# Whole expert tiles in each round of the loop, a wait for hT_hi first in the second product, and one quarter of a weight split moved from GpSimd to VectorE

## The chip, the cores and the metric

The kernel runs on one core of one Trainium2 chip. The metric is the device time of one execution in microseconds (us), the median of several runs; lower is better.

## The reference

Three layers follow one another, all in float32, on 4 batches of 576 tokens with 512 features.

```python
attn = softmax_d(q) @ (softmax_s(k)^T @ v)          # linear attention, 8 heads of 64
u    = x + (relu(x^T @ w_tok1) @ w_tok2)^T          # token mixer, 576 -> 256 -> 576
x1   = u + relu(u @ w_ch1) @ w_ch2                  # channel mixer, 512 -> 1536 -> 512
e[s] = argmax(x1[s] @ w_gate) if s == 0 or sigmoid(x1[s] @ w_local) < 0.5 else e[s-1]
out[s] = p[e[s]] * (relu(x1[s] @ w1[e[s]]) @ w2[e[s]])   # one of 8 experts, 512 -> 1024 -> 512
```

`p` is the softmax over the eight gate logits.

## The kernel before

**Products.** Every large product is made of three: a float32 matrix is kept as a high part (float32r) and a low part (raw minus high), and TensorE adds high x high, high x low and low x high into one PSUM bank (`SPLIT`). So weights have to be split before use: ScalarE or GpSimd writes the high part (`ACTIVATE` or `CAST`), VectorE or GpSimd subtracts it from the raw weights for the low part. The same holds for activations: ScalarE copies a PSUM bank to the high part (`u_h`, `hid_h`, `hT_h`, `xgT_h`), then VectorE subtracts (`u_l`, `hid_l`, `hT_l`, `xgT_l`).

**Front.** The order on each engine is written out by hand. TensorE warms up with small products (`keep_warm`), does attention of batch 0, then the eight tiles `u_tile(0, j)` (L603 on), each of eight products of 128x288 in bank 4 or 5; tile j waits until VectorE has finished `u_l` of tile j-2 (`u_done`). Behind them come the chunks of the channel mixer, `chunk(0, idx)`: twelve `hid` chunks and four `y` chunks for each half of the batch, with two banks in turn, so chunk idx waits for VectorE's result of chunk idx-2. In the first `hid` chunk `first_ready(j)` waits for the low part of quarter j of the first channel weights (`wc1`, four quarters of 128 rows, each split in two halves of 768 columns).

Who makes the low parts of `wc1`: VectorE quarters 0 and 2 (`split_first`, L1551, called between the `u_out` steps), GpSimd quarters 1 and 3 (L1861). The second channel weights (`wc2`, twelve pieces of 512 columns) are split by VectorE (even pieces, L1556) and GpSimd (odd pieces, L1864), ScalarE making the high parts in order (L1060).

**Experts.** The last batch's tokens are routed, and tokens are grouped by expert into tiles of 128 rows. Tiles 0 to 3 belong to the commonest expert and are written out one by one; the rest run in a loop over tiles `EARLY` (4) to `n`, with `n` known only on the chip. Of a tile t:

- GpSimd gathers its rows (`gather`), `x_turn(t)` transposes them on TensorE (four transposes, L743), ScalarE and VectorE make `xgT`.
- `hidden(t, n, half)` is twelve products of 128x512 (L803) into bank 0 or 1; ScalarE applies relu into `hs` (L1123).
- `h_turn(t, half)` is four transposes (L815) into bank 2 or 3; ScalarE makes `hT_h` (L1127) and signals `hT_hi`, VectorE makes `hT_l` (L1717) and signals `hT_done`.
- `output(t, n, half)` is twelve products (L828) into bank 5. VectorE scales the result (`yo_out`, L1728), GpSimd scatters it to the output.

A round of TensorE's loop before is `h_turn(t,0)`, `x_turn(t+1)`, `hidden(t,1)`, `output(t,0)`, `h_turn(t,1)`, `hidden(t+1,0)`, `output(t,1)`. It therefore straddles two tiles: `hidden(4,0)` stands ahead of the loop, and the last round also does `hidden` half 0 of a tile past the end. `output` waits for `hT_done` before its first product. Which slot holds a tile's weights is read in the loop (`version_of`, a load from `table`, L834).

While an expert is in use, the next expert's weights (eight units: 0 to 3 of `w1`, 4 to 7 of `w2`) are loaded by SyncE's queue and split by ScalarE (high, L1003) and VectorE (low, L1701), in places of a round that a word of bits picks (`units(..., FIRST_HALF | SECOND_HALF | AT_END | AFTER_END, ...)`).

```python
for a, x in SPLIT:                    # L827, in output: high x high, high x low, low x high
    last = pe.matmul(bank[5][:, :], hT[a][:, f, :], w2s[x][...], ...)
```

## Time and profile before

| | us |
|---|---|
| median of 3 runs | 725.35 (725.33 to 726.04) |
| profiled execution | 725.15 |
| its span, first to last instruction | 723.0 |
| TensorE products (PE), busy | 711.3 |
| TensorE weight loads (PEld), busy | 647.4 |
| VectorE (DVE), busy | 306.9 |
| ScalarE (ACT), busy | 231.8 |
| GpSimd (POOL), busy | 143.7 |

The page of the profile gives the time in which each engine works. Products overlap, and a product's end is modelled, so the starts of neighbouring products say more than their durations. "Idle before" a row is the time in which its engine had nothing to do, with the instruction that released it. Some instructions of TensorE's sequencer (PEldq) are listed as well: branches, loads into registers and address arithmetic, which run ahead of the array.

### The profile page before, as it was taken

The page shows a single profiled execution, that of the slowest core. Times are in us where ns is not written, and L with a number is a line of the kernel's source. Part 1 is how long each engine was busy: PE and PEld are TensorE (multiplying, and loading weights), DVE is VectorE, ACT ScalarE, POOL GpSimd, SP SyncE. Part 2 cuts the span into 40 slices and gives each one's busy share as a digit, 9 for nine tenths or more (in the row PEclk, how much of TensorE's full clock was granted, in tenths as well). Part 3 has the DMA queues.
Part 4 walks back from the last instruction along what each step waited for, and adds up shares of the span by engine and source line. Part 5 has one row for each costly group of instructions (what it writes and reads, how often), then busy time and mean ns, then how long its engine had stood idle before and what let it go on. Part 6 is the DMA issues. An engine that isn't in the chain of part 4 may idle for free.

```text
span 723.0 us, 14218 instructions
## 1 busy us (share of the span) xinstructions
PE 711.3 (98%) x4936; PEld 647.4 (90%) x4937; DVE 306.9 (42%) x639; ACT 231.8 (32%) x451; POOL 143.7 (20%) x174
## 2 busy tenths in 40 slices
PE   7999999999999999999999999999999999999997
PEld 7889999999999999999999999788888888888885
DVE  5775232235232235232225723785545552222631
ACT  4653142023142023142021133321536442222621
POOL 7754020002020002020000015022321312121311
PEclk9999999999999999999999999999999999999999
DMA  9952131012131012100010350114844561010000
GB/s 238 351 122 67 34 100 34 1 35 67 34 100 34 1 35 66 34 34 1 1 39 1 117 164 15 54 44 136 281 160 150 186 224 58 23 58 23 34 21 12
DMA packets 72013, 57.65 MB, mean 80 GB/s; under 512 B 54908, under 2 KB 57244, under 8 KB 71968
## 3 DMA queue, kind: packets, MB, share of 16 engines
q1 hardware_dynamic: 68448, 47.58, 22.1%
q0 software_dynamic: 3520, 9.44, 3.9%
q8 instruction: 32, 0.52, 0.3%
q14 instruction: 13, 0.11, 0.0%
HBM read 48.79 MB, written 10.31 MB: 82 GB/s over the span
## 4 chain that ended last, share of the span: by engine, by line
PE 96%; DVE 2%; POOL 0%; ACT 0%; issue 0%; POOLq 0%; DVEq 0%
PE bank L658 42%; PE bank L803 16%; PE bank L828 16%; PE bank L586 5%; PE bank L620 3%; PE bank L815 3%; PE bank L612 2%; PE bank L689 2%; PE bank L743 1%; PE bank L574 1%; PE bank L558 1%; PE bank L530 1%; PE bank L597 1%; DVE wc_l L1551 1%; PE bank L666 1%; PE bank L544 0%
## 5 line engine op out<-in xcount | busy, mean ns | idle before, releaser
L658 PE MATMUL bank<-u_h,wc_h 128*128 128x288 f32 x384 | 117.2, 305 | 0.1
L658 PE MATMUL bank<-hid_h,wc_h 128*128 128x288 f32 x384 | 115.0, 299 | 0.0
L658 PE MATMUL bank<-hid_l,wc_h 128*128 128x288 f32 x384 | 113.2, 295 | 0.0
L658 PE MATMUL bank<-u_h,wc_l 128*128 128x288 f32 x384 | 113.1, 295 | 0.0
L658 PE MATMUL bank<-u_l,wc_h 128*128 128x288 f32 x384 | 113.1, 294 | 0.0
L658 PE MATMUL bank<-hid_h,wc_l 128*128 128x288 f32 x384 | 113.1, 294 | 0.0
L803 PE MATMUL bank<-wslots,xgT_h 128*128 (+1 forms) x344 | 110.6, 402 | 0.0
L828 PE MATMUL bank<-wslots,hT_h 128*128 (+1 forms) x336 | 104.2, 391 | 0.0
L1509 DVE SCALAR_TENSOR_TENSOR hid_l<-bank,hid_h 128x288 fp32r<-128x288 f32 x96 | 43.5, 455 | 107.9 <-ACT hid_h L1009 106.7
L1009 ACT ACTIVATE hid_h<-bank 128x288 fp32r<-128x288 f32 x96 | 39.2, 409 | 113.4 <-PE bank L658 113.0
L828 PEld LDWEIGHTS bank<-wslots,hT_h 128*128 128x128 f32 x336 | 62.6, 188 | 13.3 <-DVE hT_l L1717 0.5
L658 PEld LDWEIGHTS bank<-u_h,wc_h 128*128 128x128 f32 x384 | 72.1, 188 | 1.0 <-DVE hid_l L1509 0.3
L658 PEld LDWEIGHTS bank<-u_l,wc_h 128*128 128x128 f32 x384 | 72.2, 188 | 0.1
L658 PEld LDWEIGHTS bank<-hid_h,wc_l 128*128 128x128 f32 x384 | 72.3, 188 | 0.0
L658 PEld LDWEIGHTS bank<-hid_l,wc_h 128*128 128x128 f32 x384 | 72.1, 188 | 0.1
L658 PEld LDWEIGHTS bank<-hid_h,wc_h 128*128 128x128 f32 x384 | 72.0, 188 | 0.1
L658 PEld LDWEIGHTS bank<-u_h,wc_l 128*128 128x128 f32 x384 | 72.0, 188 | 0.0
L803 PEld LDWEIGHTS bank<-wslots,xgT_h 128*128 128x128 f32 x344 | 61.4, 189 | 11.3
L803 PE MATMUL bank<-wslots,xgT_l 128*128 (+1 forms) x172 | 67.7, 394 | 0.0
L828 PE MATMUL bank<-wslots,hT_l 128*128 (+1 forms) x168 | 65.6, 391 | 0.0
L1516 DVE TENSOR_TENSOR x1T<-bank,u_h 128x288 f32<-128x288 f32 x32 | 14.6, 457 | 115.3 <-PE bank L658 115.3
L1915 POOL DMA_INDIRECT out_dram<-yo,id_out x21 | 22.8, 1084 | 172.7 <-DVE yo L1728 172.7
(270 smaller groups left out, 1055.3 us busy)
## 6 DMA issues: line engine op xcount, KB each, us to landing
w1raw<-in_moe_w_dram SPq DMA_DIRECT2D x20, 512.0 KB, 5.2
w2raw<-in_moe_w_dram SPq DMA_DIRECT2D x20, 512.0 KB, 3.6
wc_raw<-in_moe_w_ch_dram SPq DMA_DIRECT2D x8, 768.0 KB, 10.2
vb<-in_v_dram SPq DMA_DIRECT2D x32, 128.0 KB, 3.0
x_rows<-x1n SPq DMA_DIRECT2D x16, 256.0 KB
kb<-in_k_dram SPq DMA_DIRECT2D x24, 128.0 KB, 3.0
qb<-in_q_dram SPq DMA_DIRECT2D x24, 128.0 KB, 2.9
kraw<-in_k_dram SPq DMA_DIRECT2D x2, 512.0 KB, 6.4
```

The costliest lines, as they stand in the source:

```text
L586: last = pe.matmul(mix_bank(n, g)[:, c * TOK:(c + 1) * TOK], queries(n)[:, i, c * P:(c + 1) * P], wt1[:, i, :], start=(i == 0), stop=(i == ...
L612: pe.matmul(bank[4 + j % 2][:, 0:HS], kvd[:, c // CG, c % CG, :], qT[:, c // CG, c % CG, part], start=True, stop=False)
L620: last = pe.matmul(bank[4 + j % 2][:, 0:HS], h1T[a][:, m, c * P:(c + 1) * P], wt2[x][:, m, part], start=False, stop=(m == KT - 1 and (a, x ...
L658: last = pe.matmul(to, lhsT, rhs, start=(m == 0), stop=(m == len(mms) - 1))
L689: last = pe.transpose(bank[7][0:size, c * P:(c + 1) * P], x1T[:, c, at:at + size], ident[:, :])
L803: last = pe.matmul(bank[half][:, :], xgT[a][:, c, :], w1s[x][:, bass.ds(n & 1, 1), c, half * 512:(half + 1) * 512].rearrange("p a n -> p ( ...
L815: last = pe.transpose(bank[2 + half][:, c * P:(c + 1) * P], hs[:, f * P:(f + 1) * P], ident[:, :])
L828: last = pe.matmul(bank[5][:, :], hT[a][:, f, :], w2s[x][:, bass.ds(n & 1, 1), f, :].rearrange("p a n -> p (a n)"), start=(f == 0 and (a, ...
L1009: act.activation(hid[0][:, i, :], bank[idx % 2][:, 0:HS], ACT.Relu).then_inc(hid_hi, 1)
L1509: dve.scalar_tensor_tensor(out=hid[1][:, i, :], in0=psum, scalar=0.0, in1=hid[0][:, i, :], op0=ALU.max, op1=ALU.subtract).then_inc(chan_do ...
L1516: dve.tensor_tensor(x1T[:, i, :], psum, u[0][:, i, part], ALU.add).then_inc(y_sum, 1)
L1915: pool.indirect_dma_start(out=out.rearrange("b s d -> (b s) d"), out_offset=bass.IndirectOffsetOnAxis(ap=id_out[:, 0:1], axis=0), in_=yo[: ...
```

## The change

- TensorE's loop round is one whole tile: `hidden(t,0)`, five of the twelve products of `hidden(t,1)`, `h_turn(t,0)`, the other seven, the first quarter-step of `output(t,0)` (three products), `x_turn(t+1)`, `h_turn(t,1)`, the remaining nine products of `output(t,0)`, and `output(t,1)`. `hidden(4,0)` is gone from ahead of the loop, and `output(3,0,1)` is in one piece.
- `output` waits for `hT_hi` before its first product and for `hT_done` only before its third, the first that reads `hT_l`.
- ScalarE's and VectorE's rounds follow this order; the units of the next expert are dealt out differently (one before `hs_out(t,1)`, three, four or six behind `xgT_out(t+1)`, one after). VectorE's `yo_out(t)` is the last step of round t and no longer the first of the next.
- VectorE splits quarter 3 of `wc1` (halves at u tiles 4 and 5), its first two pieces of `wc2` come at tiles 6 and 7 and no longer at 4 and 6; GpSimd splits quarter 1 only, then waits until VectorE has finished its six halves, and goes on with `wc2`.
- `keep_warm` makes 68 products instead of 72. `tiles` holds one number instead of two.

```diff
             def first_ready(j):
-                if j % 2 == 0:
-                    pe.wait_ge(wc1_lo, 2 * (j // 2 + 1))
+                if j == 1:
+                    pe.wait_ge(wc1_lo_pool, 2)
                 else:
-                    pe.wait_ge(wc1_lo_pool, 2 * (j // 2 + 1))
+                    pe.wait_ge(wc1_lo, 2 * (j + 1 - int(j > 1)))
...
-            keep_warm(72)
+            keep_warm(68)
...
             def output(t, n, half, again, chunks=range(KF // 2)):
                 if chunks[0] == 0:
-                    pe.wait_ge(hT_done, 2 * t + half + 1)
+                    pe.wait_ge(hT_hi, 2 * t + half + 1)
...
                     for a, x in SPLIT:
+                        if c == 0 and (a, x) == SPLIT[-1]:
+                            pe.wait_ge(hT_done, 2 * t + half + 1)
...
-            output(3, 0, 1, True, FIRST)
+            output(3, 0, 1, True)
             pe.wait_ge(routed, 2)
-            hidden(EARLY, version_of(EARLY), 0, True)
-            output(3, 0, 1, True, SECOND)
             def tile(t, again):
                 n = version_of(t)
+                hidden(t, n, 0, again)
+                hidden(t, n, 1, again, range(TURN_AT))
                 h_turn(t, 0, again)
+                hidden(t, n, 1, again, range(TURN_AT, 3 * KD))
+                output(t, n, 0, again, (0,))
                 x_turn(t + 1)
-                hidden(t, n, 1, again)
-                output(t, n, 0, again)
                 h_turn(t, 1, again)
-                next_n = version_of(t + 1)
-                hidden(t + 1, next_n, 0, again=True)
+                output(t, n, 0, again, (1, 2, 3))
                 output(t, n, 1, again)
...
@@ scalar, tile
+                hs_out(t, 0)
                 hT_out(t, 0)
-                units(t, word, AFTER_END, (6, 7), again)
-                units(t + 1, word, FIRST_HALF, (0, 1), again)
-                units(t + 1, word, SECOND_HALF, (4, 5), again)
+                units(t, word, AFTER_END, (7,), again)
+                units(t + 1, word, FIRST_HALF, (0,), again)
                 hs_out(t, 1)
+                hT_out(t, 1)
                 xgT_out(t + 1)
-                units(t + 1, word, FIRST_HALF, (2, 3), again)
-                units(t + 1, word, SECOND_HALF, (6, 7), again)
-                hT_out(t, 1)
-                hs_out(t + 1, 0)
-                units(t + 1, word, AT_END, (4, 5), again)
+                units(t + 1, word, FIRST_HALF, (1, 2, 3), again)
+                units(t + 1, word, SECOND_HALF, (4, 5, 6, 7), again)
+                units(t + 1, word, AT_END, (4, 5, 6), again)
...
@@ vector, front
-                if j in (4, 6):
-                    split_second(j - 4)
+                if j in (4, 5):
+                    split_first(3, j - 4)
+                if j in (6, 7):
+                    split_second(2 * (j - 6))
...
@@ vector, tile
                 word = next_weights(t)
-                yo_out(before, again)
                 hT_out(t, 0)
                 units(t, word, AFTER_END, (6, 7))
-                units(t + 1, word, FIRST_HALF, (0, 1))
-                units(t + 1, word, SECOND_HALF, (4, 5))
+                units(t + 1, word, FIRST_HALF, (0,))
+                hT_out(t, 1)
                 xgT_out(t + 1)
-                units(t + 1, word, FIRST_HALF, (2, 3))
-                units(t + 1, word, SECOND_HALF, (6, 7))
-                hT_out(t, 1)
+                units(t + 1, word, FIRST_HALF, (1, 2, 3))
+                units(t + 1, word, SECOND_HALF, (4, 5, 6, 7))
                 units(t + 1, word, AT_END, (4, 5))
+                yo_out(t, again)
...
@@ gpsimd, front
-            for j in (1, 3):
-                for half in range(2):
-                    part = slice(half * CH // 2, (half + 1) * CH // 2)
-                    if j == 1:
-                        pool.wait_ge(wc1_hi_pool, 2 * j + half + 1)
-                    else:
-                        pool.wait_ge(wc1_hi, 2 * (j - 2) + half + 1)
-                    pool.tensor_tensor(wc1[1][:, j, part], wc1_raw[:, j, part], wc1[0][:, j, part], ALU.subtract).then_inc(wc1_lo_pool, 1)
+            for half in range(2):
+                part = slice(half * CH // 2, (half + 1) * CH // 2)
+                pool.wait_ge(wc1_hi_pool, 2 + half + 1)
+                pool.tensor_tensor(wc1[1][:, 1, part], wc1_raw[:, 1, part], wc1[0][:, 1, part], ALU.subtract).then_inc(wc1_lo_pool, 1)
+            pool.wait_ge(wc1_lo, 2 * (KD - 1))
```

```order
L815 MATMUL bank<-ident,hs 128x128 [waits hT_done,hs_done]
L815 MATMUL bank<-ident,hs 128x128 x3
L834 ISA
L834 TENSOR_LOAD table
L834 ISA x2
L796 REGISTER_ALU
L798 ISA [waits xgT_done]
L801 ISA [waits hs_done]
L803 REGISTER_ALU [waits w_split]
L803 ISA
L803 MATMUL bank<-wslots,xgT_h 128x512
```

After the change that load and `hidden` stand at the head of a round, right behind the branches and with no transposes between:

```order
L918 COMPARE_AND_BRANCH
L836 ISA
L836 TENSOR_LOAD table
L836 ISA x2
L796 REGISTER_ALU
L798 ISA [waits xgT_done]
L802 ISA [waits hs_done]
L803 REGISTER_ALU [waits w_split]
L803 ISA
L803 MATMUL bank<-wslots,xgT_h 128x512
```

The one load of `table` in a round is now the only one, and the first product behind it has nothing but the previous round's `output` ahead of it.

VectorE in the front, from the second half of quarter 0 of `wc1` on (`wc_l` at L1551 is `wc1`, at L1556 `wc2`), before:

```order
L1551 TENSOR_TENSOR wc_l<-wc_raw,wc_h 128x768 [waits wc1_hi_pool]
L1277 TENSOR_TENSOR u_l<-bank,u_h 128x288 [waits u_hi]
L1551 TENSOR_TENSOR wc_l<-wc_raw,wc_h 128x768 [waits wc1_hi]
L1277 TENSOR_TENSOR u_l<-bank,u_h 128x288 [waits u_hi]
L1551 TENSOR_TENSOR wc_l<-wc_raw,wc_h 128x768 [waits wc1_hi]
L1277 TENSOR_TENSOR u_l<-bank,u_h 128x288 [waits u_hi]
L1556 TENSOR_TENSOR wc_l<-wc_raw,wc_h 128x512 [waits wc2_hi]
L1277 TENSOR_TENSOR u_l<-bank,u_h 128x288 [waits u_hi] x2
L1556 TENSOR_TENSOR wc_l<-wc_raw,wc_h 128x512 [waits wc2_hi]
L1277 TENSOR_TENSOR u_l<-bank,u_h 128x288 [waits u_hi]
```

GpSimd at the same place, after the change (L1856 is quarter 1 of `wc1`, L1860 is `wc2`):

```order
L1852 CAST wc_h<-wc_raw 128x768
L1856 TENSOR_TENSOR wc_l<-wc_raw,wc_h 128x768 [waits wc1_hi_pool] x2
L1860 TENSOR_TENSOR wc_l<-wc_raw,wc_h 128x512 [waits wc2_hi,wc1_lo]
L1860 TENSOR_TENSOR wc_l<-wc_raw,wc_h 128x512 [waits wc2_hi] x3
```

VectorE gets two more halves of 768 columns between its u tiles, and GpSimd's first piece of `wc2` waits for `wc1_lo`, the count of VectorE's halves.

## Rows read from the trace of the kernel before

**Rows 1.** Page, busy time of each engine, share of the span, instructions.
```profile
PE 711.3 (98%) x4936; PEld 647.4 (90%) x4937; DVE 306.9 (42%) x639; ACT 231.8 (32%) x451; POOL 143.7 (20%) x174
```

**Rows 2.** Page, groups of instructions: count, busy us, mean ns, idle before.
```profile
L803 PE MATMUL bank<-wslots,xgT_h 128*128 (+1 forms) x344 | 110.6, 402 | 0.0
L828 PE MATMUL bank<-wslots,hT_h 128*128 (+1 forms) x336 | 104.2, 391 | 0.0
```

**Rows 3.** Timeline of PE, one round of the loop: start, us, instruction.
```profile
594.51 0.60 PE L815 MATMUL bank<-ident,hs 128*128 128x128 f32 x4
...
595.30 0.71 PE L803 MATMUL bank<-wslots,xgT_h 128*128 x2
...
595.85 0.40 PE L803 MATMUL bank<-wslots,xgT_l 128*128 x1
...
600.87 0.60 PE L815 MATMUL bank<-ident,hs 128*128 128x128 f32 x4
...
606.80 0.60 PE L815 MATMUL bank<-ident,hs 128*128 128x128 f32 x4
```

**Rows 4.** Timeline of ACT and DVE in that round.
```profile
598.34 0.60 ACT L1123 ACTIVATE hs<-bank 128x512 f32<-128x512 f32 x1 [2.60 <-PE bank L803]
...
601.50 0.60 ACT L1127 ACTIVATE hT_h<-bank 128x512 fp32r<-128x512 f32 x1 [2.07 <-PE bank L815]
...
602.14 0.69 DVE L1717 TENSOR_TENSOR hT_l<-bank,hT_h 128x512 fp32r<-128x512 f32 x1 [1.98 <-ACT hT_h L1127]
```

**Rows 5.** PE's sequencer by line, 602.9 to 608: count, ns, first and last start.
```profile
L828 PEldq FUSED_REGOPS  x8: 46/46/46, 603.0 to 604.0; - x8
...
L914 PEldq ALU_OP  x1: 32/32/32, 604.1 to 604.1; - x1
...
L834 PEldq TENSOR_LOAD <-table x1: 308/308/308, 604.8 to 604.8; - x1
...
L812 PEldq ALU_OP  x1: 36/36/36, 605.6 to 605.6; - x1
```

**Rows 6.** Timeline of ACT, a pair of weight units in the loop.
```profile
555.52 2.01 ACT L1003 ACTIVATE wslots<-w2raw 128x1024 f32 x2
```

**Rows 7.** Timeline of PE ahead of the loop, output(3,0,1).
```profile
502.26 0.40 PE L828 MATMUL bank<-wslots,hT_l 128*128 128x512 f32 x1
502.70 0.73 PE L828 MATMUL bank<-wslots,hT_h 128*128 128x512 f32 x2
```

**Rows 8.** Timeline of PE in the front, u tiles 4 to 6 and the first chunk.
```profile
34.38 0.69 PE L612 MATMUL bank<-qT,kvd 128*128 128x288 f32 x2
...
35.57 0.29 PE L620 MATMUL bank<-wt_h,h1T_l 128*128 128x288 f32 x1
36.71 0.75 PE L612 MATMUL bank<-qT,kvd 128*128 128x288 f32 x2 [0.85 <-DVE u_l L1277]
...
39.21 0.75 PE L612 MATMUL bank<-qT,kvd 128*128 128x288 f32 x2 [0.95 <-DVE u_l L1277]
...
42.27 0.30 PE L658 MATMUL bank<-u_h,wc_h 128*128 128x288 f32 x1
```

**Rows 9.** Timeline of DVE in the front.
```profile
32.83 0.95 DVE L1551 TENSOR_TENSOR wc_l<-wc_raw,wc_h 128x768 fp32r<-128x768 f32 x1
...
34.12 2.17 DVE L1551 TENSOR_TENSOR wc_l<-wc_raw,wc_h 128x768 fp32r<-128x768 f32 x1
...
41.61 0.68 DVE L1556 TENSOR_TENSOR wc_l<-wc_raw,wc_h 128x512 fp32r<-128x512 f32 x1
...
49.24 0.46 DVE L1509 SCALAR_TENSOR_TENSOR hid_l<-bank,hid_h 128x288 fp32r<-128x288 f32 x1
```

**Rows 10.** Timeline of POOL in the front.
```profile
33.24 4.74 POOL L1861 TENSOR_TENSOR wc_l<-wc_raw,wc_h 128x768 fp32r<-128x768 f32 x2 [0.88 <-ACT wc_h L1054]
...
55.22 2.56 POOL L1864 TENSOR_TENSOR wc_l<-wc_raw,wc_h 128x512 fp32r<-128x512 f32 x2
```

**Rows 11.** Timeline of POOL at attention: the second group's queries.
```profile
15.19 1.27 POOL L1821 TENSOR_TENSOR qb<-qb,qrec 128x640 f32<-128x640 f32 x1 [0.49 <-DVE qrec L1249]
```

More of the change, by code:

```diff
@@ L200, in build @@
             ending = sb(part2, "ending", [1, NTP + 1])
-            tiles = sb(part2, "tiles", [1, 2], I32)
+            tiles = sb(part2, "tiles", [1, 1], I32)
             mx = sb(part2, "mx", [P, J])
@@ L790, in _, with hidden @@
             batch(LAST, False, False)
-            def hidden(t, n, half, again, chunks=range(KD)):
-                if half == 0 and chunks[0] == 0:
+            def hidden(t, n, half, again, products=range(3 * KD)):
+                if half == 0 and products[0] == 0:
                     pe.wait_ge(xgT_done, t + 1)
-                if again and chunks[0] == 0:
+                if again and products[0] == 0:
                     pe.wait_ge(hs_done, 2 * t + half - 1)
-                for c in chunks:
-                    if half == 0:
+                for i in products:
+                    c, (a, x) = i // 3, SPLIT[i % 3]
+                    if half == 0 and i % 3 == 0:
                         pe.wait_ge(w_split, NU * n + c + 1)
-                    for a, x in SPLIT:
-                        last = pe.matmul(bank[half][:, :], xgT[a][:, c, :],
-                                         w1s[x][:, bass.ds(n & 1, 1), c, half * 512:(half + 1) * 512].rearrange("p a n -> p (a n)"),
-                                         start=(c == 0 and (a, x) == SPLIT[0]), stop=(c == KD - 1 and (a, x) == SPLIT[-1]))
-                if chunks[-1] == KD - 1:
+                    last = pe.matmul(bank[half][:, :], xgT[a][:, c, :],
+                                     w1s[x][:, bass.ds(n & 1, 1), c, half * 512:(half + 1) * 512].rearrange("p a n -> p (a n)"),
+                                     start=(i == 0), stop=(i == 3 * KD - 1))
+                if products[-1] == 3 * KD - 1:
                     last.then_inc(h_ready, 1)
@@ L1768, in _, with tile @@
             units(EARLY, word, AT_END, (4, 5))
-            def tile(before, again):
-                t = before + 1
+            yo_out(EARLY - 1, True)
+            def tile(t, again):
                 word = next_weights(t)
-                yo_out(before, again)
                 hT_out(t, 0)
                 units(t, word, AFTER_END, (6, 7))
-                units(t + 1, word, FIRST_HALF, (0, 1))
-                units(t + 1, word, SECOND_HALF, (4, 5))
+                units(t + 1, word, FIRST_HALF, (0,))
+                hT_out(t, 1)
                 xgT_out(t + 1)
-                units(t + 1, word, FIRST_HALF, (2, 3))
-                units(t + 1, word, SECOND_HALF, (6, 7))
-                hT_out(t, 1)
+                units(t + 1, word, FIRST_HALF, (1, 2, 3))
+                units(t + 1, word, SECOND_HALF, (4, 5, 6, 7))
                 units(t + 1, word, AT_END, (4, 5))
-            last = dve.value_load(tiles[0:1, 1:2], min_val=N // P - 1, max_val=NT - 1)
-            with dve.Fori(EARLY - 1, NT - 1) as before:
-                with dve.If(before < last):
-                    tile(before, again=True)
-            yo_out(last, True)
+                yo_out(t, again)
+            n = dve.value_load(tiles[0:1, 0:1], min_val=N // P, max_val=NT)
+            with dve.Fori(EARLY, NT) as t:
+                with dve.If(t < n):
+                    tile(t, again=True)
         @block.gpsimd
```

16 lines of the change are left out of this document (8 added, 8 removed).

## The prediction

> **What bounds the kernel now.** I read the page first. TensorE's products are busy for 711.3 of 723.0 us, and the next engine, VectorE, for 306.9 [rows 1]. So only two things can shorten this kernel: fewer products, or less waiting on TensorE. Then the page's groups of instructions: the first product of the experts has 344 high instructions and the second 336 [rows 2]. A tile needs 16 of each, so the second serves 21 tiles and the first 21 and a half. The half too many is `hidden(t+1,0)` of the last round, for a tile that doesn't exist. Next the timeline of a round: from one `h_turn(t,0)` at 594.51 to the next at 606.80 are 12.29 us. From the third product of `hidden` at 595.85 to the transposes at 600.87 are 22 products, so one takes 5.02 / 22 = 0.228 us; eight transposes take 0.79, and the first two products behind transposes 0.09 more than their pitch [rows 3]. 48 x 0.228 + 1.2 + 2 x 0.09 = 12.3: the round has no wait in it. So a new order has nothing to gain inside a round, and each wait that it brings in is paid in full, 17 times. Last the front, where TensorE does wait: two of its rows there have idle time ahead, 0.85 and 0.95 us, released by VectorE's `u_l` [rows 8].
>
> The profiled execution took 725.15 us (span 723.0 and 2.15 around it), 0.2 below the median of 725.35. The sum is made against 725.15, and the 0.2 is added at the end.
>
> **Part 1, a round is a whole tile.** There are 17 rounds in both kernels (tiles 4 to 20). `hidden(4,0)` moves into the loop, and the last round loses its spare half: 12 x 0.228 = 2.7 us. It lies on the path that sets the end, since `output(t,1)` comes behind it in the old order, and behind that only the last scaling and scatter, the same in both. **Gain 2.7.**
>
> The other rounds keep their 48 products, twelve transposes and two changes back to products. But the work that hides ScalarE and VectorE gets much shorter, so each cover has to be read. Times count from the transposes or the product named.
>
> - `h_turn(t,0)` needs `hs` of half 0. The twelfth product of `hidden` starts nine pitches behind the third, at 597.90, and the relu ends at 598.34 + 0.60 = 598.94 [rows 3, 4], 1.04 later. Five products of cover put the transposes at 6 x 0.228 = 1.37. Slack 0.3.
> - `output(t,0)` needs `hT_h`, which ends at 602.10, 1.23 behind its transposes at 600.87 [rows 3, 4]. Four transposes and seven products take 0.4 + 0.09 + 1.6 = 2.1. Slack 0.9. `hT_l` ends at 602.83, or 1.96 [rows 4]; the third product, the first to wait for it now, comes at 2.5. Slack 0.6.
> - `h_turn(t,1)` needs `hs` of half 1, 1.04 behind the last product's start. Three products and `x_turn` stand between: 4 x 0.228 + 0.4 = 1.3. Slack 0.3. But ScalarE may be at a weight unit: two take 2.01 us [rows 6]. A unit between `hT_out(t,0)` and `hs_out(t,1)` ends 0.2 to 0.4 after `hs_out` could start, which uses the slack up. Five rounds have one (the four with `FIRST_HALF` and the one with `AFTER_END`). Bounds 0 and 0.2 each; I take 0.06, a **loss of 0.3** in all, nearer to nothing because the slack covers most of the unit's overhang.
> - The head of the round. What is queued behind the waiting instruction matters here: TensorE's sequencer. It issues the twelve products of `output(t,1)` from 603.0 to 604.0, goes through the branches from 604.1, loads the slot at 604.8 and is ready at 605.6 [rows 5]; the array gets there at 606.80 [rows 3], 1.2 later. After the change it is held until `hT_l` of half 1, 1.96 behind `h_turn(t,1)`; ten products (0.9), branches and load (1.5) and the first product's addresses (0.3) bring it to 4.7. The array needs 0.4 + 0.09 + 21 x 0.228 = 5.3. Slack 0.6. Cost nothing, bounds 0 and 0.2 a round.
> - A change of expert. `xgT_out` on ScalarE ends about 8.8 into a round (its place is behind `hT_h` of half 1), six units of 1.0 [rows 6] bring it to 14.8, which is 2.5 into the next round, and `hs_out` is wanted there at 2.9. The worst case comes once. Nothing, if the weights have landed.
>
> **Part 2, hT_hi first.** The one place where the old wait cost anything is `output(3,0,1)`: its first product starts 0.44 behind its neighbour and not 0.23, and its first pair lasts 0.73 [rows 7] where an undisturbed pair behind a product lasts 0.6. `hT_h` is there in time by 0.7, `hT_l` for the third product too. **Gain 0.3.**
>
> **Part 3, the front.** VectorE splits half a quarter in 0.95 us with GpSimd quiet and in 2.17 while GpSimd splits quarter 3, 4.74 us for its two halves [rows 9, 10]; there are two such long halves. That is what holds `u_l` up, and with it u tiles 5, 6 and 7. Tile 4 starts at 34.38, its last product at 35.57, the next could start 0.13 later: 1.3 a tile [rows 8]. VectorE's steps for a tile, one `u_l` of 0.46 and one half of 0.95, with an overlap of 0.1, take 1.3 too. So tile 5 starts at 35.7 and not at 36.71, tile 6 at 37.0 and not 39.21, and the first chunk at 39.6 instead of 42.27 [rows 8]. **At most 2.7**, with the two added halves on VectorE counted in.
>
> Not all of it lasts. VectorE's four halves and the `u_l` between them, from 34.12 on, end near 39.0. Then it has its five pieces of `wc2` in front of it, and GpSimd, waiting for `wc1_lo`, starts its four. Before, these nine lay between 37.98 (33.24 + 4.74) [rows 10] and `hid_l` of chunk 3 at 49.24 [rows 9]; now TensorE wants that `hid_l` at 49.24 - 2.7 = 46.5. One after another the pieces take 5 x 0.65 (0.68 less overlap) [rows 9] + 4 x 1.28 (2.56 for two) [rows 10] = 8.4 us, so from 39.0 to 47.4, and a small reduction 0.2: 47.6. That is 1.6 gained. Up to chunk 12 VectorE is as full as before and hardly adds to its lead. I take **1.7**, between the bounds of 0.8 (each crowded piece also delays a `hid_l` for TensorE) and 2.7 (they overlap).
>
> The Trainium skill (SBUF — State Buffer, section "SBUF: two separate sides") says that a VectorE instruction with two SBUF inputs and a GpSimd instruction that reads SBUF lock each other out for the whole instruction. The trace agrees: 2.17 is 0.95 and the rest of a half on GpSimd. By that rule the nine pieces come one after another, as in the sum. If the engines shared the width in proportion, the pieces would overlap, and part 3 would be 2.4 or more.
>
> `keep_warm`: four small products less bring the first attention products forward, but the second group's queries are ready only at 15.19 + 1.27 = 16.46 [rows 11], and TensorE needs them there in both kernels. That wait covers what is saved. Nothing, bounds 0 and 0.2.
>
> **Sum.** -2.7 - 0.3 - 1.7 + 0.3 = -4.4 against 725.15, so 720.75; with the 0.2, **720.9**.
>
> **Rivals.**
> 1. *The front's lead is eaten* before chunk 12 by the crowd of `wc2` pieces. For it: VectorE has little idle time there to recover in. Against: the two extra halves run while GpSimd is silent. Part 3 is 0.5 or less: 722.1.
> 2. *The front keeps everything*, because the pieces overlap. Part 3 is 2.4 to 2.7: 720.1.
> 3. *The rounds stall*: one of the covers of 0.3 fails by 0.1 to 0.2 in each of 17 rounds, 1.7 to 3.4 in all: 722.6 to 724.3. For it: 0.3 is little. Against: every slack comes out positive by the rows.
> 4. *Slower than before*, at the head of the round: the sequencer, held by `hT_done`, arrives when the array has run dry, and branches, load and addresses lie bare. From (4.4 + 1.45) / 17 = 0.34 us a round the kernel is slower by over 0.2%. The head would have to take 0.9 us longer than I add up; at 0.4 a round, 727.7. For it: before, eight transposes hid those steps. Against: no single step in rows 5 is over 0.31.
> 5. *The change doesn't do what it says*: the last round still ends late, say because the scatter's queue is held by the later gather. It has 5 us of the round to spare. That would leave parts 2 and 3: 723.6.
>
> **Chances.** Forecast 0.54, rival 1 0.14, rival 2 0.12, rival 3 0.14, rival 4 0.04, rival 5 0.02. The range of 719.6 to 723.0 leaves out rivals 4 and 5 and the far half of rival 3, and reaches down to full gains in all parts (725.35 - 2.7 - 0.3 - 2.7). A difference within 0.2%, 1.45 us, is about what a measurement of this kernel can't tell from none. Faster by more: the forecast, rivals 1 and 2 and most of 3: 0.89. Within: the far end of 3 and a little of 5: 0.07. Slower: 0.04.
>
> **What would show it.** In the changed kernel, the high instructions of the first product count 336 like the second's; rounds take 12.3 us, with no idle time ahead of the `hs` transposes or at the head; `output(3,0,1)` follows its neighbour at 0.23; VectorE's halves of `wc1` take 0.95; the first chunk starts near 39.6, and `hid_l` of chunk 3 near 47.6. I am wrong if rounds are longer than 12.4, if the first chunk starts after 40.5, or if the lead at chunk 12 is under 1 or over 2.3 us.

## The result and the profile after

The kernel after takes 719.50 us, the median of six runs (719.42 to 720.24), beside 725.51 for the kernel before (six runs, 725.33 to 727.79). The ratio is 0.9911, with a 95% interval of 0.9899 to 0.9924. The profiled execution took 719.51 us with a span of 717.8, so 1.7 to 1.8 us lie outside the span, where 2.1 lay before. Against the profiled execution of before that is 5.64 us less; I had forecast 4.4. The measured time is 0.1 us below the low end of my range, and the six runs lie on both sides of that end, so which side the median fell on is luck; that the sum was short by 1.2 us is not. The direction and the mechanism of the two large parts were right.

The page, busy times, and two groups of instructions, which answer to [rows 1, 2]:

```profile
PE 706.7 (98%) x4920; PEld 644.5 (90%) x4921; DVE 307.0 (43%) x640; ACT 230.2 (32%) x450; POOL 134.0 (19%) x172
...
L830 PE MATMUL bank<-wslots,hT_h 128*128 (+1 forms) x336 | 105.9, 396 | 0.0
L803 PE MATMUL bank<-wslots,xgT_h 128*128 (+1 forms) x336 | 104.8, 393 | 0.0
```

Both products now have 336 high instructions: the half tile too many is gone. TensorE's timeline over one round (start, us, instruction), which answers to [rows 3], from the transposes of `h_turn(t,0)` to the next ones:

```profile
593.33 0.60 PE L815 MATMUL bank<-ident,hs 128*128 128x128 f32 x4
...
596.09 0.60 PE L743 MATMUL bank<-ident,xg 128*128 128x128 f32 x4
596.52 0.60 PE L815 MATMUL bank<-ident,hs 128*128 128x128 f32 x4
...
601.52 0.39 PE L830 MATMUL bank<-wslots,hT_l 128*128 x1
601.75 0.62 PE L803 MATMUL bank<-wslots,xgT_h 128*128 x2
...
605.61 0.60 PE L815 MATMUL bank<-ident,hs 128*128 128x128 f32 x4
```

605.61 - 593.33 is 12.28, and no row has idle time ahead of it; at the head of the round, 601.52 to 601.75, the pitch is 0.23 like everywhere. ScalarE in that round and, above it, in one with a weight unit ahead of `hs_out(t,1)`, which answers to [rows 4, 6]:

```profile
506.52 0.60 ACT L1126 ACTIVATE hs<-bank 128x512 f32<-128x512 f32 x1 [6.19 <-PE bank L803]
...
508.85 1.06 ACT L1006 ACTIVATE wslots<-w1raw 128x1024 f32 x1 [0.16 <-issue]
509.81 0.58 ACT L1126 ACTIVATE hs<-bank 128x512 f32<-128x512 f32 x1
...
592.39 0.60 ACT L1126 ACTIVATE hs<-bank 128x512 f32<-128x512 f32 x1 [2.64 <-PE bank L803]
593.97 0.60 ACT L1130 ACTIVATE hT_h<-bank 128x512 fp32r<-128x512 f32 x1 [0.98 <-PE bank L815]
595.60 0.60 ACT L1126 ACTIVATE hs<-bank 128x512 f32<-128x512 f32 x1 [1.03 <-PE bank L803]
```

Without a unit the second relu comes 3.21 behind the first, with one 3.29 (3.26 in the other three such rounds). The unit costs at most 0.08 of a slack of 0.3, and TensorE doesn't feel it: rounds with and without one last 12.27.

The front on TensorE, u tiles 4 to 7 and the first products of chunks 0 and 2, which answers to [rows 8]:

```profile
34.77 0.69 PE L612 MATMUL bank<-qT,kvd 128*128 128x288 f32 x2
...
36.09 0.65 PE L612 MATMUL bank<-qT,kvd 128*128 128x288 f32 x2
...
37.36 0.65 PE L612 MATMUL bank<-qT,kvd 128*128 128x288 f32 x2
...
38.65 0.65 PE L612 MATMUL bank<-qT,kvd 128*128 128x288 f32 x2
...
39.93 0.30 PE L658 MATMUL bank<-u_h,wc_h 128*128 128x288 f32 x1
...
42.96 0.29 PE L658 MATMUL bank<-u_h,wc_l 128*128 128x288 f32 x1
43.38 0.40 PE L658 MATMUL bank<-u_h,wc_h 128*128 128x288 f32 x1
```

The tiles come every 1.3 us, as forecast. From tile 4 to the first chunk are 5.16 us where before had 42.27 - 34.38 = 7.89, so 2.73 are won there. Then chunk 2 starts 0.42 and not 0.13 behind its neighbour: a part is given back. VectorE beside it, which answers to [rows 9]:

```profile
38.38 0.95 DVE L1552 TENSOR_TENSOR wc_l<-wc_raw,wc_h 128x768 fp32r<-128x768 f32 x1
39.29 0.46 DVE L1278 TENSOR_TENSOR u_l<-bank,u_h 128x288 fp32r<-128x288 f32 x1
39.67 1.58 DVE L1557 TENSOR_TENSOR wc_l<-wc_raw,wc_h 128x512 fp32r<-128x512 f32 x1
...
41.54 1.42 DVE L1557 TENSOR_TENSOR wc_l<-wc_raw,wc_h 128x512 fp32r<-128x512 f32 x1
42.88 0.44 DVE L1510 SCALAR_TENSOR_TENSOR hid_l<-bank,hid_h 128x288 fp32r<-128x288 f32 x1
...
46.64 0.68 DVE L1557 TENSOR_TENSOR wc_l<-wc_raw,wc_h 128x512 fp32r<-128x512 f32 x1
...
47.40 0.46 DVE L1510 SCALAR_TENSOR_TENSOR hid_l<-bank,hid_h 128x288 fp32r<-128x288 f32 x1
```

The halves of `wc1` take 0.95. Four of the five `wc2` pieces meet GpSimd's and take 1.40 to 1.58 instead of 0.68, and `hid_l` of chunk 3 comes at 47.40 (forecast 47.6, before 49.24).

GpSimd's scaling of the second group's queries, 15.19 before [rows 11], is later in this execution:

```profile
15.56 1.26 POOL L1820 TENSOR_TENSOR qb<-qb,qrec 128x640 f32<-128x640 f32 x1 [0.49 <-DVE qrec L1250]
```

Between these two executions the whole front is 0.4 later as well: u tile 4 at 34.77 and not 34.38.

**Where the 5.64 us are.** I cut both traces at the same events of TensorE. The logit transposes are L537 in both, 51.76 before and 50.04 after; `h_turn(3,1)` starts at 500.24 and 498.61; the cut called "hidden(4,0) and output(3,0,1) done" lies at 508.30 (the loop's first transposes) and 506.32 (twelve products behind 503.60); the last product starts at 717.26 and 711.98, and the spans, to two places, are 723.04 and 717.75.

| stretch | before | after | difference |
|---|---|---|---|
| start of the span to u tile 3 | 33.10 | 33.48 | +0.38 |
| to the first logit transposes of the next batch | 18.66 | 16.56 | -2.10 |
| to h_turn(3,1) | 448.48 | 448.57 | +0.09 |
| to hidden(4,0) and output(3,0,1) done | 8.06 | 7.71 | -0.35 |
| to the last product | 208.96 | 205.66 | -3.30 |
| to the end of the span | 5.78 | 5.77 | -0.01 |
| outside the span | 2.11 | 1.76 | -0.35 |

The -3.30 is the spare half, 2.73, and 0.57 from shorter rounds: from `hs` of tile 5 to `hs` of tile 20 are 15 rounds, 184.60 us before (518.08 to 702.68) and 184.10 after (518.75 to 702.85), so 12.307 and 12.273 each.

### The profile page after: what moved, and what is told of

It is laid out like the page before. It is cut to its first block, busy times and chain, and to the rows that moved or that the text cites. A ratio compares the mean times of both kernels' runs of the same rounds, so it can differ in the third digit from the quotient of the medians.

```text
span 717.8 us, 14035 instructions
## 1 busy us (share of the span) xinstructions
PE 706.7 (98%) x4920; PEld 644.5 (90%) x4921; DVE 307.0 (43%) x640; ACT 230.2 (32%) x450; POOL 134.0 (19%) x172
## 4 chain that ended last, share of the span: by engine, by line
PE 92%; SPq 3%; DVE 2%; DMA 1%; POOL 1%; ACT 1%; issue 0%; POOLq 0%; DVEq 0%
PE bank L658 40%; PE bank L803 16%; PE bank L830 16%; PE bank L586 4%; PE bank L620 3%; PE bank L815 3%; SPq L388 2%; PE bank L689 2%; PE bank L612 2%; PE bank L743 1%; PE bank L558 1%; PE bank L574 1%; PE bank L597 1%; POOL qb L1820 1%; PE bank L666 1%; DMA qraw<-in_q_dram 1%
## 5 line engine op out<-in xcount | busy, mean ns | idle before, releaser
L830 PE MATMUL bank<-wslots,hT_h 128*128 (+1 forms) x336 | 105.9, 396 | 0.0
L803 PE MATMUL bank<-wslots,xgT_h 128*128 (+1 forms) x336 | 104.8, 393 | 0.0
L1719 DVE TENSOR_TENSOR hT_l<-bank,hT_h 128x512 fp32r<-128x512 f32 x42 | 29.0, 692 | 95.3 <-ACT hT_h L1130 94.9
```

The source lines that it names most:

```text
L803: last = pe.matmul(bank[half][:, :], xgT[a][:, c, :], w1s[x][:, bass.ds(n & 1, 1), c, half * 512:(half + 1) * 512].rearrange("p a n -> p ( ...
L830: last = pe.matmul(bank[5][:, :], hT[a][:, f, :], w2s[x][:, bass.ds(n & 1, 1), f, :].rearrange("p a n -> p (a n)"), start=(f == 0 and (a, ...
L1719: dve.tensor_tensor(hT[1][:, part, :].rearrange("p c n -> p (c n)"), bank[2 + half][:, :], hT[0][:, part, :].rearrange("p c n -> p (c n)") ...
```

## The experiments

Four things were open: whether the front is worth 1.7 or 2.0; what part 2 does, and where; how thin the covers in a round really are; why 0.35 us outside the span went, for which I had no term; and whether the 0.35 ahead of the loop are really what part 2 gave. The runs in one table. "Outside" is the time outside the span over all of a kernel's runs (their spans are known to 0.1 us, so each value to 0.05), "front" the stretch from u tile 3 to the first logit transposes, "round" the mean of 15 or 16 rounds by ScalarE's `hs`, "length" the number of instructions in VectorE's program, a loop's counted once.

| kernel | median us | ratio to before, 95% | outside | front | round | length |
|---|---|---|---|---|---|---|
| before | 725.35 to 725.98 | | 2.06 to 2.16 | 18.66 | 12.31 | 706 |
| after | 719.50 | 0.9911 (0.9899, 0.9924) | 1.66 to 1.74 | 16.56 | 12.27 | 703 |
| e1 before again | 725.90 | 1.0004 (0.9995, 1.0013) | 2.07 to 2.16 | 18.59 | 12.31 | 706 |
| e2 front only | 722.95 | 0.9963 (0.9949, 0.9977) | 1.70 to 1.78 | 16.55 | 12.31 | 708 |
| e3 loop only | 721.56 | 0.9943 (0.9929, 0.9957) | 1.69 to 1.80 | 18.58 | 12.27 | 701 |
| e4 keep_warm 72 | 719.85 | 0.9916 (0.9903, 0.9930) | 1.67 to 1.75 | 16.56 | 12.27 | 703 |
| e5 hT_done first | 724.09 | 0.9973 (0.9961, 0.9984) | 1.69 to 1.73 | | 12.53 | 703 |
| e6 transposes at 3 | 722.90 | 0.9962 (0.9948, 0.9976) | 1.66 to 1.76 | | 12.50 | 703 |
| e7 two units | 722.84 | 0.9962 (0.9948, 0.9976) | 1.70 to 1.78 | | 12.27, four of 13.0 | 703 |
| e8 before plus 3 | 725.03 | 0.9987 (0.9977, 0.9996) | 1.77 to 1.86 | | 12.31 | 709 |
| e9 nine on VectorE | 720.04 | 0.9919 (0.9907, 0.9932) | 2.10 to 2.15 | 15.93 | 12.27 | 707 |
| e10 GpSimd behind 5 | 720.96 | 0.9929 (0.9917, 0.9942) | 1.68 to 1.74 | 17.72 | 12.27 | 703 |
| e11 GpSimd free | 719.48 | 0.9911 (0.9896, 0.9925) | 1.67 to 1.71 | 16.47 | 12.27 | 703 |
| e12 after plus 3 | 719.53 | 0.9910 (0.9895, 0.9924) | 2.05 to 2.13 | 16.56 | 12.27 | 706 |
| e13 nine plus 1 | 719.20 | 0.9905 (0.9890, 0.9921) | 1.69 to 1.74 | 15.92 | 12.27 | 708 |
| e14 nine plus 6 | 719.17 | 0.9909 (0.9896, 0.9923) | 1.67 to 1.76 | 15.92 | 12.27 | 713 |
| e15 before plus 1 | 725.43 | 0.9992 (0.9983, 1.0002) | 2.10 to 2.16 | | 12.31 | 707 |
| e16 after plus 5 | 719.62 | 0.9912 (0.9897, 0.9927) | 1.69 to 1.76 | 16.54 | 12.27 | 708 |

### The two halves of the change

**e1, before again.** No edit. 

> The kernel before, unchanged, as a run of its own. Two things are asked of it: the part of an execution that lies outside the span (2.15 us in the profiled execution of before, 1.7 to 1.75 in all six of the kernel after), and the second group's queries in attention (GpSimd's scaling at 15.19 before, 15.56 after). Theory A: both differ from execution to execution; then this kernel's executions spread over 1.7 to 2.2 us outside the span. Theory B: both belong to the change; then this kernel stays at 2.1 to 2.2 and at 15.2. Ratio 1.000.

Half of each theory. The 2.1 outside the span are constant: all 11 runs of it and all 15 of before beside it lie at 2.06 to 2.16, so they belong to the program. The late queries don't: here they come at 15.42. Over all eighteen profiles GpSimd's scaling starts anywhere between 15.10 and 16.91 and u tile 3 between 33.10 and 34.13 (35.68 once), and the one does not settle the other: e12 has 15.10 and 33.53, before 15.19 and 33.10. The profile of before that I read was the earliest of all in u tile 3. The 0.38 us that after lost there is within this spread.

**e2, front only.** Before, with the three edits of the front.

> The kernel before with part 3 of the change alone (VectorE splits quarter 3, GpSimd waits for wc1_lo), keep_warm at 72. Theory A (the gains add): the first chunk starts 2.7 us earlier than in the kernel before where attention ends at the same time, hid_l of chunk 3 at 47.0 to 47.4, the lead at chunk 12 is 2.0, the kernel 2.0 faster than before (723.4). Theory B (the front was sized rightly at 1.7 and the late attention of the kernel after has nothing to do with it): 723.7 to 723.9. Theory C (the lead is eaten later): under 0.8 faster.

**e3, loop only.** After, with these three undone and `keep_warm` at 72.

> The kernel after with the front as before (part 3 undone, keep_warm at 72); parts 1 and 2 stay. Theory A (the miss is in the rounds): 2.7 for the spare half, 0.3 for the wait on hT_hi, 0.6 for rounds of 12.27 instead of 12.29 to 12.35, so 3.6 faster than before (721.8), rounds at 12.27. Theory B (rounds cost the same as before, and the miss is the time outside the span): 3.0 faster, 722.4, with 1.7 us outside the span. Theory C (the unit rounds stall by what I forecast): 2.7 faster.

e2: Theory A. From tile 3 to the logit transposes it takes 16.55 us, after 16.56, the two kernels with the old front 18.59 and 18.58: the front is worth 2.0 to 2.1, in either surrounding. It came out at 722.95, 2.65 under the median beside it and not 2.0, and two things that have nothing to do with the front make the rest: 1.75 outside the span, and no gap ahead of `output(3,0,1)`. e3: Theory A too, rounds of 12.27 in the new order whatever the front is, and 721.56 for 721.8.

**e4, keep_warm at 72.**

```diff
-            keep_warm(68)
+            keep_warm(72)
```

> The kernel after with 72 small products at the start instead of 68. Theory A (the wait for the second group's queries covers them): same time as after within 0.1, 719.5. Theory B (the four fewer products are why attention came 0.4 later): 0.4 faster, 719.1, and GpSimd's scaling of the second group's queries at 15.2 and not 15.56.

u tile 3 starts at 33.96, not earlier, the queries are scaled at 15.38, and the median is 0.35 higher, within what attention's start varies by (spans 717.3 to 718.6). No gain from 72, so Theory B finds no support; my "nothing" for the four products stands as far as this can tell.

### Part 2 works in another place than I thought

**e5, hT_done first.**

```diff
                 if chunks[0] == 0:
-                    pe.wait_ge(hT_hi, 2 * t + half + 1)
+                    pe.wait_ge(hT_done, 2 * t + half + 1)
```

> The kernel after with part 2 undone: output waits for hT_done before its first product, as in before. Theory A (my part 2): the first product of output(3,0,1) again starts 0.44 behind its neighbour and the kernel loses 0.3, 719.8. Theory B (the gap was VectorE's late start of hT_l of tile 3, at 501.95 when hT_h was written at 501.47, which the kernel with the front change alone has not, though it still waits for hT_done first): hT_l starts within 0.15 of hT_h's end, no gap, 719.5. In the rounds hT_l of half 0 ends at 595.29 and output(t,0) starts at 595.40, so neither theory expects a cost there; if there is one it is up to 0.1 x 17.

B was right on the gap and both were wrong on the rounds: 4.6 us slower than after, three quarters of the whole gain of the change. `output(3,0,1)` runs at its pitch without part 2. But in the loop, the last product of `hidden` and the first of `output(t,0)`, TensorE, then VectorE:

```profile
509.85 0.39 PE L803 MATMUL bank<-wslots,xgT_l 128*128 x1
510.23 0.72 PE L830 MATMUL bank<-wslots,hT_h 128*128 x2
510.79 0.39 PE L830 MATMUL bank<-wslots,hT_l 128*128 x1
...
509.31 0.69 DVE L1719 TENSOR_TENSOR hT_l<-bank,hT_h 128x512 fp32r<-128x512 f32 x1 [4.17 <-ACT hT_h L1130]
```

and what the sequencer does in between (count, ns, first and last start):

```profile
L826 PEldq ALU_OP  x1: 32/32/32, 510.0 to 510.0; - x1
...
L830 PEldq FUSED_REGOPS  x2: 46/46/46, 510.1 to 510.3; - x2
L830 PEld LDWEIGHTS bank<-wslots,hT_h x2: 186/186/187, 510.2 to 510.3; 128*128 128x128 f32 x2
```

`hT_l` ends at 510.00, `output` would be due at 509.85 + 0.23 = 510.08, so I had read a slack of 0.1. But the wait stands in the sequencer ahead of the reckoning of the slot's address (`ALU_OP` at 510.0, `FUSED_REGOPS` at 510.1, the weight load at 510.2), and the product starts 0.23 behind `hT_l`. The pitch is 0.38 instead of 0.23, and the pair lasts 0.10 longer: 0.25 a round, 4.3 in 17. In the kernel before, the first product of `output(3,0,1)`, behind the gap, has a constant address, and the product at 502.70 starts only 0.06 behind `hT_l` (501.95 + 0.69). With `hT_hi` first, the wait is over long before, the addresses are reckoned ahead, and the late wait falls on the third product.

### How thin the covers are

**e6, the transposes behind three products instead of five.**

```diff
-            TURN_AT = 3 * KD // 2 - 1
+            TURN_AT = 3
```

> The kernel after with three products of hidden(t,1) ahead of h_turn(t,0) instead of five. The relu ends at 592.99 and the transposes start at 593.33, a slack of 0.34; two products less take 0.45. Theory A (slack as read, a wait is paid in full in each round): idle time of 0.11 to 0.2 ahead of the transposes, rounds of 12.4 to 12.5, the kernel 2 to 3.4 slower than after, 721.5 to 722.9. Theory B (TensorE's work in flight hides it): 719.5.

Theory A: rounds of 12.50, 3.4 slower than after. ScalarE's relu of half 0 and what follows it on TensorE:

```profile
594.07 0.60 ACT L1126 ACTIVATE hs<-bank 128x512 f32<-128x512 f32 x1 [2.65 <-PE bank L803]
594.33 0.39 PE L803 MATMUL bank<-wslots,xgT_l 128*128 x1
594.73 0.66 PE L815 MATMUL bank<-ident,hs 128*128 128x128 f32 x4
```

Relu's end is 594.67, the transposes, whose addresses are constant, follow 0.06 later; their pitch is 0.40 instead of 0.23, and the rest of the 0.23 lost in a round is in the transposes themselves and the products behind them.

**e7, two units ahead of hs_out(t,1).**

```diff
                 units(t, word, AFTER_END, (7,), again)
-                units(t + 1, word, FIRST_HALF, (0,), again)
+                units(t + 1, word, FIRST_HALF, (0, 1), again)
                 hs_out(t, 1)
...
-                units(t + 1, word, FIRST_HALF, (1, 2, 3), again)
+                units(t + 1, word, FIRST_HALF, (2, 3), again)
```

> The kernel after with two weight units on ScalarE ahead of hs_out(t,1) in the four rounds with FIRST_HALF instead of one. One unit delays hs by 0.04 (509.81 against 506.52 + 3.20 + 0.05) and not by the 0.2 to 0.4 that I took. Theory A (slack of 0.3 as read, a second unit costs 0.96 more): 0.65 to 0.7 in each of four rounds, 2.6 to 2.8 slower than after, 722.1 to 722.3. Theory B (half of it is hidden again): under 1.5.

Theory A, and a little more: the first of the four rounds takes 13.09 (506.18 to 519.27), the others 13.02 to 13.04, so about 0.8 each and 3.3 in all by the medians. TensorE waits for `hs` with nothing else to do:

```profile
509.85 0.60 PE L743 MATMUL bank<-ident,xg 128*128 128x128 f32 x4
511.05 0.66 PE L815 MATMUL bank<-ident,hs 128*128 128x128 f32 x4 [0.60 <-ACT hs L1126]
```

So one unit costs nothing and two cost 0.8 a round: my 0.06 for one was the wrong side of the edge.

### The crowd of wc2 pieces

In after, VectorE and GpSimd split pieces of `wc2` at the same time and stretch each other's. Three runs deal that work out differently.

**e9, the first nine pieces on VectorE** (ten of the twelve in all).

```diff
-        BY_VECTOR = (0, 2, 4, 6, 8, 10)
-        BY_POOL = (1, 3, 5, 7, 9, 11)
+        BY_VECTOR = (0, 1, 2, 3, 4, 5, 6, 7, 8, 10)
+        BY_POOL = (9, 11)
...
-                if j in (6, 7):
-                    split_second(2 * (j - 6))
+                if j == 6:
+                    split_second(0)
+                    split_second(1)
+                if j == 7:
+                    split_second(2)
...
                 chunk_out(0, idx)
+                split_second(3 + 2 * idx)
                 split_second(4 + 2 * idx)
```

> The kernel after with VectorE splitting the first nine pieces of wc2 (three between u tiles, two behind each of the first three hid_l) and GpSimd only pieces 9 and 11. Theory A (VectorE's and GpSimd's pieces go one after another, so four pieces of 1.28 on GpSimd are replaced by four of 0.65 on VectorE; hid_l of the first chunks is no longer late): VectorE's pieces take 0.68 each, TensorE does not pause at chunks 2 to 4, hid_l of chunk 3 at about 46.6 instead of 47.40 (for a u tile 3 at 33.48), and from tile 3 to the first logit transposes 15.9 to 16.2 instead of 16.56: 0.3 to 0.6 faster than after. Theory B (the engines overlap, VectorE now has more to do): 0 to 0.5 slower.

**e10, GpSimd waits for VectorE's fifth piece of wc2.**

```diff
-            pool.wait_ge(wc1_lo, 2 * (KD - 1))
+            pool.wait_ge(wc2_lo, 5)
```

> The kernel after with GpSimd's first piece of wc2 waiting for VectorE's fifth piece (wc2_lo at 5) instead of its six halves of wc1. Theory A (one after another): VectorE's five pieces take 0.68, hid_l of chunk 3 about 0.8 earlier, but kmax and lgp of the next batch, two SBUF inputs each, now meet GpSimd's pieces and take 1.3 instead of 0.68 and 0.43; from tile 3 to the first logit transposes 16.0 to 16.5, at chunk 12 nothing gained: within 0.3 of after. Theory B (the crowd costs nothing beyond itself): the same time to 0.1.

**e11, GpSimd doesn't wait.** The same line taken out.

> The kernel after without GpSimd's wait for wc1_lo. Its first piece of wc2 can start at 37.2, when ScalarE has written the high part, and the second at 39.8. Theory A (one after another): VectorE's half of wc1 at 37.10 or 38.38 takes 2.0 to 2.2 instead of 0.95, u tiles 6 and 7 are late by 1.0, the first chunk at 40.9 instead of 39.93, but the pieces behind it are less crowded: 0 to 0.6 slower than after. Theory B (they overlap): 0.1 to 0.3 faster, since GpSimd is done earlier.

e9 by Theory A: 15.93 in the front, 0.63 less than after, with no pause at a chunk. VectorE of e9:

```profile
42.51 1.28 DVE L1557 TENSOR_TENSOR wc_l<-wc_raw,wc_h 128x512 fp32r<-128x512 f32 x2
43.72 0.46 DVE L1510 SCALAR_TENSOR_TENSOR hid_l<-bank,hid_h 128x288 fp32r<-128x288 f32 x1
```

Two pieces alone take 1.28, less than one took beside GpSimd. Yet the median is 720.04: the time outside the span has gone from 1.7 to 2.1, see below.

e10 has the first half of Theory A (pieces of 0.68, `hid_l` on time) and pays more than forecast for the second, 1.5 us by the medians instead of at most 0.3. VectorE of e10, and TensorE's logit transposes:

```profile
46.97 1.03 DVE L1195 TENSOR_TENSOR kmax<-kb 128x512 f32<-128x512 f32 x1
48.04 1.40 DVE L1198 TENSOR_TENSOR lgp<-kmax 128x256 f32<-128x256 f32 x1
49.47 1.37 DVE L1201 TENSOR_TENSOR lgp<-lgp,kb 64x256 f32<-64x256 f32 x1
50.77 0.44 DVE L1510 SCALAR_TENSOR_TENSOR hid_l<-bank,hid_h 128x288 fp32r<-128x288 f32 x1
...
50.90 0.44 PE L537 MATMUL bank<-ident,lgp 128*128 128x128 f32 x2 [1.62 <-DVE lgp L1201]
```

The two `lgp` steps, 0.43 and 0.42 in e9 and after, take 1.40 and 1.37, as long as one of GpSimd's pieces (5.83 for four), and TensorE waits for them with 1.62 idle. I had seen the collision and not that `kmax` and the two `lgp` stand on the path. The Trainium skill (SBUF — State Buffer, section "SBUF: two separate sides") says that the loser of the two engines blocks for the other's whole instruction, and that a VectorE instruction takes part only if it has two SBUF inputs or runs in a mode that uses both ports. The trace agrees as far as it goes: `lgp`, with two SBUF inputs and 256 columns, stretches by about 1, less than a whole piece, while `hid_l` at 50.77, with one input in PSUM, keeps its 0.44 beside a GpSimd piece.

e11 comes out as after, 719.48 for 719.50. One half of `wc1` is stretched:

```profile
38.54 1.64 DVE L1552 TENSOR_TENSOR wc_l<-wc_raw,wc_h 128x768 fp32r<-128x768 f32 x1
```

That is the collision of Theory A, but shorter than its 2.0 to 2.2, and nothing on TensorE's path comes late by it: the first chunk comes 6.44 behind tile 3, in after 6.45, where Theory A had it a whole microsecond later. Theory B's gain did not come either. So GpSimd's new wait is worth nothing here; what the front gains comes from quarter 3 being on VectorE.

### Where VectorE's instructions lie

**e8, before plus 3.**

```diff
             for b in range(1, LAST):
                 batch(b, True, True)
+            for i in range(3):
+                dve.memset(filler[0:1, i:i + 1], 0.0)
             batch(LAST, False, False)
```

> The kernel before with three tiny memsets of an unused tile on VectorE ahead of the last batch, nothing else. Asked is whether the place of the instructions in VectorE's program matters. Theory A (it does): hT_l of tile 3 half 1 starts right behind hT_h and the gap of 0.3 ahead of output(3,0,1) goes, or the time outside the span falls from 2.1 to 1.7, so 0.3 to 0.7 faster than before. Theory B (it doesn't): gap and 2.1 stay, same time, 725.6 to 725.9.

Theory A, in both its signs: three instructions that do nothing of use make the kernel 0.9 us faster by the medians (ratio 0.9987, its interval below 1). VectorE and ScalarE at tile 3, half 1. Before, its `hT_h` and `hT_l`:

```profile
500.87 0.60 ACT L1127 ACTIVATE hT_h<-bank 128x512 fp32r<-128x512 f32 x1 [1.20 <-PE bank L815]
501.95 0.69 DVE L1717 TENSOR_TENSOR hT_l<-bank,hT_h 128x512 fp32r<-128x512 f32 x1 [2.02 <-ACT hT_h L1127]
```

and with the three memsets:

```profile
501.71 0.60 ACT L1127 ACTIVATE hT_h<-bank 128x512 fp32r<-128x512 f32 x1 [1.20 <-PE bank L815]
502.44 0.69 DVE L1719 TENSOR_TENSOR hT_l<-bank,hT_h 128x512 fp32r<-128x512 f32 x1 [1.66 <-ACT hT_h L1127]
```

Before, VectorE starts 0.48 behind the end of `hT_h` with nothing to wait for, here 0.13. That 0.35 was the gap ahead of `output(3,0,1)`.

**e12, after plus 3.** The same memsets in the kernel after. 

> The kernel after with the same three memsets on VectorE that made the kernel before 0.9 faster. Theory A (they only move VectorE's instructions off a bad place, which the kernel after does not have: hT_l starts 0.13 behind hT_h, 1.7 us lie outside the span): same time as after, within 0.2. Theory B (they are worth something anywhere, or the place can be made worse): another time outside the span, or the gap of 0.3 at output(3,0,1).

Theory B in part: no gap, but 2.1 outside the span. The spans of its four runs (717.3 to 717.7) lie below those of after (717.7 to 718.5) by less than the start of the front varies, so that the median hides the 0.4.

So far the programs with 706 and 707 instructions on VectorE were the ones with 2.1. Four runs asked for that alone: **e13** and **e14**, nine pieces plus one and plus six memsets, **e15**, before plus one, **e16**, after plus five.

> The kernel with nine pieces on VectorE and one tiny memset on VectorE more, 708 instructions of its program instead of 707. Theory A (the time outside the span hangs on the length of VectorE's program, and 706 and 707 are the bad ones): 1.75 outside the span instead of 2.1, median 719.2 to 719.7 or less, 0.4 less than with 707. Theory B (the 2.1 belongs to the nine pieces or to the memsets themselves): 2.1, same time as with 707.

> The same with six memsets, 713 instructions. Theory A: 1.7 to 1.85 outside the span, unless the bad lengths come back in a pattern that I don't know. Theory B: 2.1. The span, where attention ends at the same time, is the same as in the kernel with nine pieces to 0.1 in both.

> The kernel before with one memset on VectorE, 707 instructions. Theory A for the time outside the span: 2.1, as with 706. The gap ahead of output(3,0,1) is another matter: either it hangs on the exact place of one instruction in VectorE's program (then it may go: hT_l 0.13 behind hT_h, span 0.3 shorter), or on the same lengths (then it stays).

> The kernel after with five memsets on VectorE, 708 instructions. Theory A: 1.75 outside the span, same time as after (719.5), though two memsets fewer or more (706) give 2.1. Theory B (memsets cost 0.4 at the end): 2.1, 719.9.

All four as Theory A has it: 1.7 with 708 and 713, 2.1 with 707. In e15 the gap goes though the 2.1 stay (`hT_l` at 504.20, `hT_h` done at 504.07), so these are two effects. Kernels of the same length agree in the time outside, whatever else they hold (706: before and e12; 707: e9 and e15; 708: e2, e13 and e16). What in the length does it, I can't show; other engines' programs differ too between these kernels, but in e8, e12 and e13 to e16 against their parents only VectorE's does.

The best kernel is the one with nine pieces and a length off 707, 719.17 and 719.20. Its front is 0.64 shorter than that of after. By the medians it is 0.3 faster than after, and the intervals overlap.

## Why the prediction was right or wrong

The forecast failed in its sum, and three terms made most of the miss of 1.24 us: the length of a round was carried over unchanged (0.57), so was the time outside the span (0.35), and a loss was put in that did not come (0.3). The front, part 3, was sized too small by another 0.4. Each is taken up below.

**The bound.** Right: TensorE was the only engine that counted, in both kernels.

**Part 1, 2.7 for the spare half.** Measured 2.73. The covers held: nothing waits in a round. For the head of the round I had forecast 0.6 of slack. The sequencer's rows of after, which answer to [rows 5] (count, ns, first and last start):

```profile
L836 PEldq TENSOR_LOAD <-table x1: 311/311/311, 600.2 to 600.2; - x1
L836 PEldq SEQ_ASSERT  x1: 18/18/18, 600.7 to 600.7; - x1
```

The slot is known at 600.7, and the first product's addresses, which my 0.6 included, stand in this row:

```profile
L803 PEldq FUSED_REGOPS  x1: 51/51/51, 601.2 to 601.2; - x1
```

They are done at 601.25, 4.7 behind `h_turn(t,1)` at 596.52 as forecast, and the array arrives at 601.75: a slack of 0.5.

**Part 1, "a loss of 0.3" for the five unit rounds.** Wrong: measured 0. I let the unit end 0.2 to 0.4 after the relu could start, and my own rows don't give that: behind the transposes of `h_turn(t,0)` the unit ends at 1.23 + 1.0 = 2.2; the last product starts at 1.9 and the relu 0.44 behind it, at 2.3. Measured, the unit delays it by 0.05 to 0.08. And I held it for gradual, where it is an edge: one unit costs nothing, a second 0.8 (e7).

**Part 1, "the other rounds keep their 48 products".** They do, but not their length: 12.273 for 12.307, 0.57 in all. That a new order has nothing to gain inside a round was a step that failed; I rounded both to 12.3. Reversing the order (e2, e3) shows that it goes with the loop. Behind each change from transposes to products the pitch is 0.230 to 0.233 for a while, then 0.227; in before's round that lasts for all the products of a `hidden`, in after's it stops sooner. Some of before's rounds have 0.05 more (12.35). Why, in both cases, is open.

**Part 2, 0.3 at output(3,0,1).** The 0.3 were measured, and the reason was wrong. That gap was VectorE's late start and goes without part 2 (e2, e5, e8, e15). Part 2's real work is in the loop, where it saves 4.6 us that the new order would have cost (e5). My step "slack 0.6" for the third product holds (`hT_l` done at 595.29, the product at 595.86); that there was none for a wait at the first product, I hadn't asked, since I priced part 2 by the old order alone.

**Part 3, 1.7 between 0.8 and 2.7.** Mis-sized: 2.0 to 2.1 in e2 and after. The first chunk was right (2.7 won up to it). The nine `wc2` pieces, by my sum 8.4 us one after another, take 7.65 (39.67 to 47.32 on VectorE): GpSimd's run on beside `hid_l` and `u_l`, which lie in the same stretch and which such a piece doesn't hold up. The late attention, 0.38, hid most of this, 0.4 of 0.6, so that `hid_l` of chunk 3 looked as forecast (47.40 for 47.6) and for the wrong reason.

**"Span 723.0 and 2.15 around it".** I carried the 2.15 over unchanged. It is the program's own, but goes with the length of VectorE's program, which the change shortened from 706 to 703: 0.35 less between the two profiles, 0.4 over all runs. The missing 1.24 is then 0.3 for the loss that did not come, 0.57 for the rounds, 0.35 here, 0.4 for the front and 0.1 for parts 1 and 2 together, less the 0.38 of the late attention and 0.1 lost in small pieces.

**The range** reached down "to full gains in all parts" and left no room for gains outside the parts. Rivals 1 and 3 to 5 did not come; rival 2 (the front keeps 2.4 to 2.7) was nearer than I gave it credit for. Rival 3 was close, though: the same change with the old wait (e5), or with the transposes two products earlier (e6), stalls in every round and is 3.4 to 4.6 slower. Rival 4 was not: the head of the round has 0.5 to spare, as forecast.

## What to carry to other kernels

When an order is changed so that covers get thin, read the slack not to the end of the producer but to the start of the consumer behind a wait, with what the sequencer must still reckon there: here 0.06 us with a constant address (e6, e7), 0.23 with one from a register (e5). Put a wait at the first instruction that needs the data, not at the head of the group. Before a few tenths of a microsecond are put down to an edit, change the length of a program by an instruction or two that do nothing; here that alone moved the time outside the span by 0.3 to 0.4 us and the medians by up to 0.9.

## What the runs showed that I had not expected

- The time outside the span is 2.05 to 2.16 us with 706 or 707 instructions in VectorE's program (before, e1, e9, e12, e15) and 1.66 to 1.86 with 701, 703, 708, 709 and 713 (the thirteen others), each constant to about 0.1 over its runs. The cause is open.
- One VectorE instruction started 0.35 late with nothing to wait for, in both profiles of the kernel before; with one instruction more ahead of it (e15) it did not.
- The start of u tile 3 varies from 33.10 to 34.13 us between profiled executions, 35.68 in one; a difference of half a microsecond in the first 35 us of this kernel says nothing of an edit.
